# The filter perceptron's inner product of a long-convolution kernel: one full-height product with a zero-padded weight, or two half-height products

## The reference, cut to what matters

```python
# attention-like part: x, v (12480, 128), pos_emb (12480, 64), w1 (64, 64), w2 (64, 128)
h_mlp = np.maximum(pos_emb @ w1, 0.0) @ w2
h_filt = h_mlp * np.exp(-0.01 * pos)[:, None]
y = irfft(rfft(x * v, 2 * S) * rfft(h_filt, 2 * S), 2 * S)[:S]
a = x * y
# then two feed-forward layers, 128 -> 2048 -> 128 each
b = np.maximum(a @ w_in1, 0) ** 2 @ w_out1
out = prelu(b @ w_in2, alpha) @ w_out2
```

## Time and profile before

| what | value |
|---|---|
| time before, median of 3 runs | 1385.48 us (1385.04 to 1386.36) |
| the profiled execution's own time | 1383.66 us |
| its span | 1381.8 us |
| TensorE busy (matmul) | 1368.9 us, 99% of the span |
| VectorE busy | 1118.5 us, 81% |
| ScalarE busy | 1122.3 us, 81% |
| GpSimd busy | 180.0 us, 13% |
| perceptron's inner layer on TensorE (line 741) | 128 matmul records, from 3.73 to 18.90 us |

### The profile page before, as it was taken

The page is one execution under the profiler, slowest core; times in us unless marked ns, Lnnn a source line. Parts: engine busy times, 40 slices in busy tenths (PEclk is TensorE's granted clock), DMA queues, the critical chain, the costliest instruction groups (busy, mean ns, idle before and its releaser), DMA issues.

```text
span 1381.8 us, 19839 instructions
## 1 busy us (share of the span) xinstructions
PE 1368.9 (99%) x6879; PEld 1155.9 (84%) x6879; DVE 1118.5 (81%) x1399; ACT 1122.3 (81%) x1504; POOL 180.0 (13%) x202
## 2 busy tenths in 40 slices
PE   9999999899999999999999999999999999999998
PEld 8988888898888888888888888888888888888887
DVE  6888889468778878887888788887888878888888
ACT  3778888258778877887888888888888888888887
POOL 4547888410000000000000000000000000000000
PEclk9999999999999999999999999999999999999999
DMA  8538897520010110000000000000000000000000
GB/s 268 176 118 255 275 284 222 171 90 1 28 32 1 31 32 13 27 0 9 8 8 8 0 9 8 8 0 8 9 8 8 0 8 9 8 8 0 9 9 15
DMA packets 53587, 75.35 MB, mean 55 GB/s; under 512 B 5357, under 2 KB 37587, under 8 KB 53507
## 3 DMA queue, kind: packets, MB, share of 16 engines
q1 hardware_dynamic: 46995, 64.24, 14.8%
q10 hardware_dynamic: 6384, 9.99, 2.4%
q0 software_dynamic: 128, 0.02, 0.0%
HBM read 54.93 MB, written 19.23 MB: 54 GB/s over the span
## 4 chain that ended last, share of the span: by engine, by line
PE 94%; DVE 2%; ACT 2%; DMA 1%; issue 1%; SPq 0%; POOL 0%; ACTq 0%; DVEq 0%
PE ps L188 13%; PE ps L190 13%; PE ps L189 13%; PE ps L203 12%; PE ps L205 12%; PE ps L204 12%; PE ps L758 5%; PE ps L795 3%; PE ps L874 3%; PE ps L773 3%; PE ps L781 2%; PE ps L766 1%; PE ps L741 1%; DVE stage L398 1%; PE ps L842 1%
## 5 line engine op out<-in xcount | busy, mean ns | idle before, releaser
L412 DVE TENSOR_TENSOR g_lo<-stage,g_hi 128x1024 fp32r<-128x1024 f32 (+2 forms) x199 | 238.2, 1197 | 165.3 <-ACT g_hi L313 164.7
L188 PE MATMUL ps<-x_hi,w_hi 128*128 128x512 f32 (+2 forms) x800 | 310.7, 388 | 0.5 <-DVE x_lo L382 0.3
L203 PE MATMUL ps<-g_hi,w_hi 128*128 128x512 f32 (+2 forms) x800 | 309.1, 386 | 2.0 <-DVE g_lo L444 1.4
L190 PE MATMUL ps<-x_lo,w_hi 128*128 128x512 f32 (+2 forms) x800 | 307.7, 385 | 0.0
L189 PE MATMUL ps<-x_hi,w_lo 128*128 128x512 f32 (+2 forms) x800 | 307.6, 385 | 0.0
L205 PE MATMUL ps<-g_lo,w_hi 128*128 128x512 f32 (+2 forms) x800 | 307.5, 384 | 0.0
L204 PE MATMUL ps<-g_hi,w_lo 128*128 128x512 f32 (+2 forms) x800 | 307.4, 384 | 0.0
L322 ACT ACTIVATE relu<-ps 128x1024 f32<-128x1024 f32 (+2 forms) x200 | 201.6, 1008 | 111.2 <-PE ps L190 108.4
L398 DVE SCALAR_TENSOR_TENSOR stage<-stage,alpha_sb 128x512 f32<-128x512 f32 (+2 forms) x400 | 276.2, 732 | 0.4 <-ACT stage L355 0.2
L355 ACT ACTIVATE stage<-ps,sign_sb 128x512 f32<-128x512 f32 (+2 forms) x400 | 250.9, 672 | 2.3 <-PE ps L190 1.0
L444 DVE TENSOR_TENSOR g_lo<-g,g_hi 128x1024 fp32r<-128x1024 f32 (+2 forms) x200 | 239.0, 1195 | 12.9 <-ACT g_hi L343 12.8
(11 more groups left out here) (68 smaller groups left out, 1217.8 us busy)
## 6 DMA issues: line engine op xcount, KB each, us to landing
g_dram<-work SPq DMA_DIRECT2D x49, 256.0 KB, 3.5
work<-dft_back SPq DMA_DIRECT2D x66, 128.0 KB, 3.2
gt<-g_dram SPq DMA_DIRECT2D x10, 784.0 KB
gt<-x_seq SPq DMA_DIRECT2D x32, 196.0 KB
work<-v_seq SPq DMA_DIRECT2D x32, 196.0 KB
work<-dft_forward SPq DMA_DIRECT2D x49, 128.0 KB, 3.4
x<-x_gate ACTq DMA_DIRECT2D x16, 390.0 KB, 4.6
out_t<-x SPq DMA_DIRECT2D x23, 256.0 KB, 2.0
```

The source lines that it names most:

```text
L188: nc.tensor.matmul(into[:, c, :t], w_hi[k][:, at], x_hi[layer][:, :t], start=True, stop=False)
L190: last = nc.tensor.matmul(into[:, c, :t], w_hi[k][:, at], x_lo[layer][:, :t], start=False, stop=True)
L203: nc.tensor.matmul(acc[layer][:, :t], w_hi[k][:, at], hi[:, c], start=first, stop=False)
L412: nc.vector.tensor_tensor(lo[:, :, :t], g2[at][:, :, :t], hi[:, :, :t].bitcast(FP32), ALU.subtract).then_inc(g2_lo_ready, 1)
```

## The change

Each product of 128 rows and 128 moving columns becomes two: rows 0 to 63 (block 0) at tile position (0, 0), and rows 64 to 127 (block 1) at (64, 0), both with the same 98 weight columns and with the 64 moving columns of the `w1` in their own corner. The corners with zeros are no longer read. The two products of a slice go into different PSUM banks: a fill's first bank now holds block 0 and its second bank block 1, with eight slices of 64 results in each. VectorE's two instructions per fill stay; their view of PSUM changes from "slice, half, output" to "half, slice, output", so each reads one bank where it read halves of two. Nothing else changes: loads, waits, counts of semaphores and order are the same.

```diff
--- before.py
+++ after.py
@@ mlp_fill
                 at = slice((8 * i + n) * R, (8 * i + n + 1) * R)
-                last = nc.tensor.matmul(two_banks(i % 4)[:R, n * P:(n + 1) * P], pos_sb[:, at], w1_sb,
-                                        start=True, stop=True)
+                for half in range(2):
+                    last = nc.tensor.matmul(ps[:R, 2 * (i % 4) + half, n * HID:(n + 1) * HID], pos_sb[HALF[half], at],
+                                            w1_sb[HALF[half], HALF[half]], start=True, stop=True,
+                                            tile_position=(N1 * half, 0))
             last.then_inc(mlp_done, 1)
@@ window_fill
-            src = two_banks(i % 4)[:R, :].rearrange("p (n h o) -> p h o n", n=8, h=2)
+            src = two_banks(i % 4)[:R, :].rearrange("p (h n o) -> p h o n", n=8, h=2)
```

## The result

The changed kernel takes 1388.22 us in the median of 17 executions (1385.63 to 1395.27), the kernel before 1385.43 us in the median of 17 taken beside them (1383.47 to 1387.48). The ratio is 1.0027, 95% interval 1.0017 to 1.0038: slower by 0.27%, where 0.12% faster was forecast, and outside the forecast range of 1382.4 to 1386.0.

The account below looks back on a forecast made before the run. TensorE was taken to bound the kernel: the inner layer ends 2.9 us earlier, 1.5 are given back, chunk 1's stall of 0.35 goes, 1.6 taken; from 1385.48 that gives 1383.9 us, range 1382.4 to 1386.0.

Parts of the forecast that it names:

- What bounds the kernel, and the order of the waits: Whole kernel: TensorE busy 99% of the span; after the shortened inner layer, the wait for the first u takes over.
- By TensorE alone: Inner layer: bound by TensorE alone, each VectorE fill of 1.29 us following 0.46 us of waiting for TensorE.
- Halves side by side: Inner layer: two half-height records run beside each other and cost what one full-height record does, 0.110 us at 128 columns.
- The pass at 2.4 GHz: Inner layer: one upper and one lower half-height record together take 0.085 us at full clock, near the weight load's time.
- A: Rival, inner layer: a pass still costs 0.110 us as at line 781, time 1385.5 to 1385.8; chance 0.14.
- B: Rival, inner layer: TensorE can't be fed so many instructions, no gain from 0.058 us a record, 1387.8 or 1396.8; chance 0.11.
- End of the inner layer: 14 passes done by 5.70 us, 114 more at 0.085; the layer ends near 16 us against 18.90.
- Rival C: Clock: shifted half-clock stretch, 1.7 us either way, or 1.2 GHz for longer, some 5 us lost; chances 0.08 gain, 0.03 loss.
- C's other thought: Before stage 1's chunk 0: the idle microsecond could leave the clock at 1.2 GHz longer, some 5 us lost if through 10.
- The gain of the quick executions: Stage 1's start: 2.9 us saved in the layer, 1.5 given back, chunk 1's stall of 0.35 gone; 1.6 taken.
- the time of the first u: Stage 1's chunk 0: GpSimd starts the first u at 15.87 and has it ready at 17.18, so chunk 0 starts at 17.2.
- nothing behind it is tied to an absolute time: Behind stage 1's start: TensorE sets the pace and loads move along, so the gain of 1.6 us carries to the end.

Follow-up runs that it names:

- experiment 1: The changed kernel once more, no edit, with a profile of a quick execution: 1386.11 us median of 12, ratio 1.0011.
- experiment 9: Changed kernel with the 64 moving columns streamed twice in the first two fills only: 1385.18 us median of 11, ratio 1.0000.
- the second of the four: Second of four more profiles of the changed kernel, no edit: 1385.12 us.
- experiment 2: Changed kernel with 14 warm-up matmuls ahead of the layer in place of 7: 1385.30 us median of 10, ratio 0.9998.
- experiment 3: Changed kernel with full-height products of 64 moving columns, one after the other, in place of half-height pairs: 1394.95 us median of 4, ratio 1.0059.
- experiment 5: Changed kernel with 1 warm-up matmul in place of 7: 1394.03 us median of 4, ratio 1.0050.
- the mixed variant: The kernel of experiment 9: changed kernel, moving columns streamed twice in the first two fills only; 1385.18 us, ratio 1.0000.
- experiment 7: Changed kernel with full-height products of 64 moving columns and 1 warm-up matmul in place of 7: 1414.79 us median of 4, ratio 1.0200.
- experiment 6: Changed kernel with the 64 moving columns streamed twice and 1 warm-up matmul in place of 7: 1386.15 us median of 10, ratio 1.0002.
- experiment 10: The mixed variant with the first x and v loaded ahead of the last three pieces of `pos_sb`: 1388.96 us median of 12, ratio 1.0022.
- first of the four profiles: First of four more profiles of the changed kernel, no edit: 1394.67 us.

## Why the prediction was wrong, point by point

**What bounds the kernel, and the order of the waits: right in the main.** The layer is bound by TensorE, and when it is quick, the first u takes over (1.11 and 1.78 us of waiting in experiments 1 and 9). "By TensorE alone" was too much: in the second profile of the kernel before the layer waited 0.26 us for a piece of `pos_sb`, and in two quick profiles of the change 0.26 us (experiment 1) and 0.53 us (the second of the four). The end of the quick layer, put at 16, was 16.9 and 17.5.

**Halves side by side: right.** Experiments 2 and 3 give 0.086 us for two half-height records and for one of full height. Entering half height cost 0.13 us (first record at 3.86 in experiment 1, at 3.73 in experiment 3 and before), within the 0.33 allowed for it. VectorE's two instructions stayed at 1.29 us, as costed.

**The pass at 2.4 GHz: right,** 0.086 for 0.085. A, 0.110, and B, a limit of instructions, fall: 511 weight loads and matmuls went through in 11.00 us, 0.043 us a pair of them, less than B's 0.058. (The 9.3 us that the prediction works out beside its 9.7 is 0.4 less and not 0.3; nothing hangs on it.)

**The step that failed** is in "End of the inner layer": "Up to 5.70 some 14 passes are done (...). The other 114 at 0.085 take 9.7 us". It took the rise of the clock at 5.70 over from the kernel before, as if it were a time and not an answer to what TensorE does. Of the six profiles of the changed kernel three show no rise until stage 1 has begun, and one a rise that does not last; these four are of the late group, ten of 33 executions, and experiment 5 makes all executions such. In them the layer takes up to 128 passes at 0.167 us: 21.4 us instead of the 12.3 forecast (13.0 in experiment 1). The price follows from the rows after: +7.0 us at stage 1's start and +2.0 until the clock is up, 9 us in all against the first profile of the kernel before. The late group's mean, 1394.1, is 8.7 above the median of the kernel before. What makes the clock rise in time in one execution and not in the next, with the same 7 warm-up matmuls ahead, stays open.

**Rival C had the mechanism, at half its price.** It said that products with half the moving columns could leave the clock at 1.2 GHz, gave that 10 us, a loss of 5 from the forecast of 1383.9 and a chance of 0.03; the late group lies 10.2 above 1383.9. The rows had more: line 741's weight load of 98 columns lasts up to 289 ns at the lower clock and 166 in the median at the upper, and its pace halves with the clock. A pass bound by its weight load would then be twice 0.085 (measured: 0.167), 12 and not 14 of them are done by 5.70, and as nothing in the rows said that the layer would end the slow time, it had to be costed through all 128 passes. Of the 17 timed executions five lie in the late group and six in the middle one; that moves the median by more than the whole gain. C's other thought, that the idle microsecond before chunk 0 keeps the clock down, is not borne out: it stayed up behind waits of 1.11 and 1.78 us there.

**The gain of the quick executions was too high, 1.6 us.** Against the second profile of before, whose first matmul of line 758 starts at 19.06, the profile of experiment 1 starts stage 1 1.05 us earlier and is 1.3 us ahead at chunk 1's end; the mixed variant 0.3 and 0.5. (Against the first profile, where that matmul is at 18.72, they are 0.7 and 1.0 for experiment 1, and nothing for the mixed variant's start.) The term mis-sized is the time of the first u, 17.2 by one profile: GpSimd began at 15.87 there, at 16.60 and 17.38 in the other two. And of the 1.3 us nothing was left at 200 us in experiment 1: TensorE waited 3.2 us for `dft_forward` between 86 and 262 us, against 1.0 in the second profile of before. That "nothing behind it is tied to an absolute time" is left open: the second of the four profiles was still 1.1 us ahead of the second profile of before at 248 us, but level with the first. Single executions lose more to such waits than the gain. Whether an earlier start makes them likelier was not tried.

**The comparison with one profile.** The span of 1381.8 was 2.1 below the second profile of the same kernel. The predicted time was made from the median and was not harmed by that.

## What to carry to other kernels

When a change makes each matmul do less, so that its weight load sets the pace, read the clock as part of the price: cost the stretch at both levels, and ask which of the products ahead of it and in it have so far come with a rise. Cutting the zeros out of a product saved 0.023 us a pass and took away what lifted the clock. Leave the product wide where another wait (here the first u, ready at 17.1 to 18.7) takes most of the gain anyway; wide products first had no late execution in 11, but no gain either. And look at more than the median, since two groups of executions 8 us apart were visible in the list of times before any trace was read.

## What the runs showed of the hardware that was not expected

- TensorE with a matmul record in flight for 42.45 us without a break stayed at 1.2 GHz with 64 moving columns per product and 98 weight columns (experiment 7). The Trainium skill ("TensorE: Matmul & The Clock Gate", What's actually happening) says that "activity releases the throttle", by how busy TensorE has recently been; here 42.45 us of what the profile counts as 100% busy came with no rise, while the half-height pairs streamed twice came with one at 8.4 us, 4.5 us after they began (experiment 6).
- The stream of float32 weight loads goes by TensorE's clock: a pass with 98 weight columns costs 0.086 us at 2.4 GHz and 0.167 at 1.2 (read as the weight load's time, see experiment 3). The Trainium skill (the same page, LDWEIGHTS) gives P/1.2 ns for P columns, 82 for 98, without a level; that agrees at 2.4 GHz and is half of what was measured at 1.2.
- Two half-height weight loads and matmuls take the time of one of each at full height, for 256 records in a row and not only in bursts of 16.
- In two profiles a wait within the narrow layer was followed by a fall of the clock: 1.11 us of waiting, and the fall 0.8 us after it (first of the four profiles); 2.24 us, and the fall 2.3 us after it (experiment 10). Waits of 1.11 and 1.78 us ahead of stage 1's wide products were not followed by one (experiments 1 and 9).
